# Batch 0's channel product by seven half products too, with w_ch1's quadrants and w_ch2's sums made at other places

## The reference

```
x   = softmax(rot(q) @ rot(k).T / 8) @ v           # heads side by side: 576 x 512 per batch
h   = relu(x.T @ w_tok1) @ w_tok2                  # w_tok1 576 x 256, w_tok2 256 x 576
u   = x + h.T
out = u + relu(u @ w_ch1) @ w_ch2                  # w_ch1 512 x 1536, w_ch2 1536 x 512
```

## Time and profile before

| | |
|---|---|
| time, median of 3 runs | 640.83 us (640.73 to 640.95) |
| profiled execution: span from its first to its last instruction | 639.1 us |
| profiled execution: granted PE clock, mean | 0.998 of full |
| u units of batch 0 begin | at 298.9 us |
| w_ch1 product of batch 0 begins | at 308.6 us |
| u units of batches 1 and 2 begin | at 388.9 and 472.9 us |

### The profile page before, as it was taken

How to read it: one execution, slowest core, us unless ns; L and a number is a source line. 1 busy time by engine, 2 the same in 40 slices (tenths; PEclk the granted TensorE clock), 3 DMA queues, 4 the chain that set the end, 5 groups by cost and what they waited for, 6 DMA issues and landing times.

```text
span 639.1 us, 13808 instructions
## 1 busy us (share of the span) xinstructions
PE 621.5 (97%) x4724; PEld 604.7 (95%) x4724; DVE 509.4 (80%) x877; ACT 464.2 (73%) x1016; POOL 341.0 (53%) x316
## 2 busy tenths in 40 slices
PE   3899999999999999999999999999999999999997
PEld 3799999999999999999999999999999999999997
DVE  6899999999999999987385985569935499553895
ACT  3889999988889899986383664776556765567753
POOL 3999999998888887560900002860017800068200
PEclk9999999999999999999999999999999999999999
DMA  4767766767668774406001332000320002100002
GB/s 133 168 159 197 212 151 179 187 173 183 174 176 211 203 189 114 122 20 216 19 1 44 155 84 75 1 2 2 84 74 0 0 0 80 43 33 1 1 3 74
DMA packets 61898, 63.01 MB, mean 99 GB/s; under 512 B 18896, under 2 KB 46160, under 8 KB 61840
## 3 DMA queue, kind: packets, MB, share of 16 engines
q1 hardware_dynamic: 61392, 62.15, 35.7%
q10 hardware_dynamic: 448, 0.10, 0.1%
HBM read 31.46 MB, written 9.44 MB: 64 GB/s over the span
## 4 chain that ended last, share of the span: by engine, by line
PE 95%; SPq 1%; DVE 1%; DMA 1%; ACT 0%; issue 0%; ACTq 0%; DVEq 0%
PE slot L615 12%; PE rest L648 12%; PE rest L625 9%; PE slot L1344 8%; PE slot L1346 8%; PE slot L1345 8%; PE rest L1344 6%; PE rest L1346 6%; PE rest L1345 6%; PE rest L376 3%; PE rest L576 3%; PE rest L635 2%; PE slot L1376 2%; PE rest L1376 2%; PE rest L224 1%; PE rest L221 1%
## 5 line engine op out<-in xcount | busy, mean ns | idle before, releaser
L1335 POOL TENSOR_TENSOR w_ch_part<-w_ch_sums,w_ch_part 128x512 fp32r<-128x512 f32 x21 | 31.0, 1474 | 173.3 <-ACT w_ch_part L1588 173.3
L984 DVE TENSOR_REDUCE neg_max<-slot 128x1 f32<-128x576 f32 x142 | 106.7, 752 | 6.6 <-PE slot L615 2.2
L1652 ACT ACTIVATE pieces<-h 128x288 fp32r<-128x288 f32 x168 | 73.8, 444 | 49.8 <-PE slot L1346 25.3
L992 DVE TENSOR_TENSOR pt_lo<-rest,pt_hi 128x512 fp32r<-128x512 f32 x144 | 96.0, 677 | 1.9 <-ACT pt_hi L845 1.3
L648 PE MATMUL rest<-pt_hi,v 128*128 128x256 f32 (+1 forms) x320 | 89.3, 303 | 0.0
L845 ACT ACTIVATE pt_hi<-rest 128x512 fp32r<-128x512 f32 x144 | 84.1, 595 | 5.2 <-PE rest L625 4.3
L1743 DVE TENSOR_TENSOR pieces<-h,pieces 128x288 fp32r<-128x288 f32 x168 | 74.6, 454 | 9.4 <-ACT pieces L1652 8.9
L648 PE MATMUL rest<-pt_lo,v 128*128 128x256 f32 (+1 forms) x256 | 69.7, 295 | 0.0
L615 PE MATMUL slot<-key,q_hi 128*128 128x288 f32 x252 | 63.5, 333 | 2.2 <-ACT prob_a L838 1.0
L838 ACT ACTIVATE prob_a<-slot,neg_max 128x576 f32<-128x576 f32 x78 | 58.0, 743 | 10.1 <-DVE neg_max L984 10.0
L648 PEld LDWEIGHTS rest<-pt_hi,v 128*128 128x128 f32 x320 | 60.3, 188 | 0.1
(11 more groups left out here) (263 smaller groups left out, 2107.3 us busy)
## 6 DMA issues: line engine op xcount, KB each, us to landing
key<-t_hi_k SPq DMA_DIRECT2D x31, 144.0 KB, 2.3
key<-t_lo_k SPq DMA_DIRECT2D x31, 144.0 KB, 2.4
raw_qk<-in_q_dram SPq DMA_DIRECT2D x16, 256.0 KB, 2.8
raw_v<-in_v_dram SPq DMA_DIRECT2D x16, 256.0 KB, 3.3
x_scratch<-x_pair SPq DMA_DIRECT2D x16, 256.0 KB, 2.1
stage_or_x<-x_scratch SPq DMA_DIRECT2D x16, 256.0 KB, 4.3
q_hi<-t_hi_q SPq DMA_DIRECT2D x31, 128.0 KB, 2.4
q_cross<-t_hi_q SPq DMA_DIRECT2D x31, 128.0 KB, 2.4
```

Source lines behind the costliest of these rows:

```text
L984: dve.tensor_reduce(neg_max[p % 2][:, i:i + 1], slot[g if 2 <= g < 4 else g % 2][:, :, 0:HALF], AX.XY, ALU.max, negate=True).then_inc(maxe ...
L992: dve.tensor_tensor(pt_lo[:, :, cols], rest[:, bank, :].rearrange("p (j n) -> p j n", j=G), f32(pt_hi[:, 0:G, cols]), ALU.subtract).then_i ...
L1652: act.activation(pieces[:, ring(m), 0, :], source[WEIGHTS[n]][:, ft, :], ACT.Copy).then_inc(piece_hi, 1)
```

## The change

1. Batch 0 uses the seven half products as the other batches do. `hidden`, `hidden_out`, `u_hi`, `u_lo`, `add_u` and the special order of `t1` and `t3` in batch 0 go.
2. w_ch1 is loaded once, by the same eight DMAs, into the places of the quadrants. It is no longer split as a whole. POOL makes the sum S1 and then S3 in late attention (p = 14 and 15), DVE makes S2 at its end and S4 in batch 0. The four loads and the four sums in batch 0's channel stage go.
3. w_ch2's sums move from POOL to DVE, between the steps of the half products; `w2_hi(n)` stands on ACT behind each half product n; of the lo parts, DVE makes numbers 0 and 1 and POOL numbers 2 to 6, behind its 21 ring rests.

The diff, cut to its core:

```diff
 class ChannelWeights:
+    def load(self, sp, w_ch1, n, c):
+        name, c0, col = (("S3", 0, 1), ("A22", CT // 2, 1), ("A11", 0, 0), ("A12", CT // 2, 0))[n]
+        sp.dma_start(self.share[name][:, c, :],
+                     w_ch1[(c0 + c) * P:(c0 + c + 1) * P, col * CH // 2:(col + 1) * CH // 2]).then_inc(self.loaded, 16)
+    def early_sum(self, pool, n):
+        out, x, y, op = (("S1", "S3", "A22", ALU.add), ("S3", "A11", "S3", ALU.subtract))[n]
...
+    def late_sum(self, dve, n):
+        out, x, y = (("S2", "S1", "A11"), ("S4", "A12", "S2"))[n]
...
+        dve.tensor_tensor(self.share[out], self.share[x], self.share[y], ALU.subtract).then_inc(self.late_sums, 1)
# attention, POOL (p = 14, 15) and the end of DVE's list; ACT's eight w1.split_hi go
-                w1.split_lo(pool, p - (N - 2))
+                w1.early_sum(pool, p - (N - 2))
-        w1.split_lo(dve, 2)
+        w1.late_sum(dve, 0)
# mixer, POOL
-        weight_sum("S1", "A21", "A22", ALU.add)
...
+        for k in range(HIDDEN):
+            ring_rest(0, k)
+        for n in range(W2_FIRST, len(WEIGHTS)):      # W2_FIRST = 2
+            w2_lo(n)
# mixer, PE
-                for j in range(PLAIN):
-                    hidden(j)
+            for n in range(len(SHARES)):
+                for i in range(PAIR):
+                    shared(b, n, i)
...
+            if begins and n < W2_FIRST:
+                pe.wait_ge(w2_lo_first, n + 1)
+            elif begins:
+                pe.wait_ge(w2_lo_then, n - W2_FIRST + 1)
# mixer, ACT: ring_part, and shares
+            elif k == 2 and begins:
+                act.wait_ge(x_stored, 48 * PAIRS)
...
+            if k == PAIR and begins:
+                act.wait_ge(w1.early_sums, 2)
+                act.wait_ge(w1.late_sums, 2)
...
                 if n + 2 < len(SHARES):
                     share_part(b, n + 2)
+                if begins:
+                    w2_hi(n)
...
+        ring_part(0, 0, begins=True)
         body(0, begins=True)
# mixer, DVE: shares, and the start of batch 0
             share_rest(b, 2)
+            if begins:
+                w2_sums(0)
+                w2_sums(1)
             for i in range(PAIR):
                 keep(b, i)
+            if begins:
+                w2_sums(2)
             share_rest(b, 3)
+            if begins:
+                w2_sums(3)
             share_rest(b, 4)
+            if begins:
+                w2_lo(0)
             share_rest(b, 5)
...
             share_rest(b, 6)
+            if begins:
+                w2_lo(1)
...
+                first.last_sums(dve)
+                w1.late_sum(dve, 1)
+            shares(b, begins)
```

More of the change, by code:

```diff
@@ L112, in build @@
         with ExitStack() as ctx:
-            then = mixer(nc, ctx, sb, slot, ident, h, h1, pieces, token, wt2, wc1, w1, w1_sums, w1_parts, h_early, x_stored, first, w_ch1, w_ch2,
+            then = mixer(nc, ctx, sb, slot, ident, h, h1, pieces, token, wt2, w1, w1_parts, h_early, x_stored, first, w_ch1, w_ch2,
                          out)
@@ L143 @@
 Mixer = namedtuple("Mixer", "sync gpsimd tensor scalar vector first_token_hi")
+SHARES = ("A11", "S2", "S3", "A22", "A12", "S1", "S4")
 class ChannelWeights:
[L149 to L170, removed]
+    def __init__(self, nc, whole, sums):
+        self.share = {name: sums[:, n] for n, name in enumerate(SHARES)}
+        self.loaded, self.early_sums, self.late_sums = (whole.enter_context(nc.semaphore(f"w_ch1_{n}"))
+                                                        for n in ("loaded", "early_sums", "late_sums"))
@@ L1238, in mixer, with t_count @@
     last_columns = sem("last_columns")
[L1240 to L1245, removed]
+    def t_count(b, which, f):
+        return b * TS + (which - 1) * HF + f + 1
     def used(b, n):
@@ L1279, in sync, with body @@
         sp.dma_start(w2_whole["A21"][:], w[:, top, HC * P:DM]).then_inc(w_in, 16)
[L1281 to L1290, removed]
+        def body(b, last=False):
             if not last:
@@ L1378, in u_unit @@
             mm.then_inc(unit_ready, 1)
[L1380 to L1392, removed]
-                    mm = products(s[:, g, 0:HALF], [w[:, c, ft * P:(ft + 1) * P] for w in wc1],
-                                  [x[:, c, f * HALF:(f + 1) * HALF] for x in ut], c == 0, c == CT - 1)
-            mm.then_inc(unit_ready, 1 if j < PLAIN - 1 else 1 + HIDDEN - PLAIN)
         def shared(b, n, i):
@@ new lines, in body @@
+                first.last_sums(dve)
+                w1.late_sum(dve, 1)
+            shares(b, begins)
+            lo(b, 3)
+            t1(b, 0)
+            lo(b, 4)
+            t1(b, 1)
+            t1(b, 2)
+            lo(b, 5)
+            for f in range(3, HF):
+                t1(b, f)
+                lo(b, 3 + f)
+            for f in range(HF):
+                t2(b, f)
+                lo(b, 9 + f)
+            for f in range(HF):
+                t3(b, f)
+                lo(b, 15 + f)
```

264 lines of the change are left out of this document (78 added, 186 removed).

## The result

The changed kernel takes **663.05 us** (median of five runs, 662.6 to 664.3) where the kernel before takes 640.90 (640.73 to 641.32) beside it: a ratio of **1.0347**, 95% interval 1.0335 to 1.0358, so slower by 3.5%. The forecast was 665.7, with a range of 648 to 672. The profiled execution took 664.3 us, with a span of 662.5; its forecast was 665.7 and 664. A second measurement of the same kernel, in another job, gave 664.33 with a span of 662.4. Two variants of different jobs can therefore differ by some 1.3 us without a cause in the kernel. Two executions far outside the rest, one of 873.82 us of the variant *spread* and one of 2175.91 of the kernel before, are left out everywhere.

What follows compares the result with a forecast made beforehand. PE was taken to bound the kernel, busy 97% of the span and throughout batch 0. The terms -4.8 + 0.8 + 5.0 + 4.0 + 2.15 + 15.9 + 1.8 = +24.9 on 640.83 gave 665.7 us, range 648 to 672.

Steps and rivals of the forecast that it cites:

- Matmuls, -4.8: Batch 0: 36 fewer matmuls at 0.133 us each save 4.8 us.
- Start, +0.8: Start of batch 0: DVE's late w_ch1 sum delays the last normalisation, the store of x and unit 3: +0.8 us.
- Sums in front of keep, +5.0: Before unit 6: two w_ch2 sums on DVE, alternating with POOL's rests, delay DVE's copy of S2: +5.0 us.
- ACT before w2_hi(1), +4.0: Before unit 9: ACT's split of S1 waits for all four w_ch2 sums, holding ring part 9 behind it: +4.0 us.
- Units 12 and 18, 2.15: Later half products: added splits and lo parts delay ring part 12 and POOL's rests; unit 12 waits 1.25, unit 18 0.9 us.
- POOL's five, +15.9: Channel product: POOL's five w_ch2 lo subtractions alternate with DVE's instructions on the shared port, making DVE's lo's late: +15.9 us.
- my 0.4 each: Within POOL's five lo subtractions: 0.4 us for each of four DVE turns, added to 5 x 3.5 us.
- Clock, +1.8: Channel product: after a long wait PE runs at half pace for 3.5 us, once, losing 1.8 us.
- (a): Rival: the stalls are hidden and only the saved matmuls count, 636.0 us; needs keep 0 in time; 5%.
- (b): Rival, channel product: POOL's long subtractions stop DVE's short ones little or not at all, 649.0 us; 18%.
- (c): Rival, channel product: DVE, queued back to back, keeps the port; POOL enters only at gaps; 18.2 for 15.9, so 668; 8%.
- (d): Rival: the clock stays low through the channel product, +23, about 688 us; 4%.

Runs made afterwards that it cites:

- spread: Changed kernel with ACT's splits one half product later, w_ch2's sums and w_ch1's S4 standing apart, all seven lo parts on DVE: 650.91 us, ratio 1.0159.
- the last kernel: Changed kernel without w_ch2's four sums, its seven lo parts written as zeros, POOL's memsets behind DVE's last max: 640.12 us, ratio 0.9985.
- S4 later: Changed kernel with DVE's sum S4 of w_ch1 moved from in front of the share sums to behind w2_lo(0): 664.64 us, ratio 1.0369.
- Splits later: Changed kernel with ACT's splits of w_ch2, except number 0, one half product later: 661.44 us, ratio 1.0321.
- POOL only writes: Changed kernel with POOL's five lo subtractions replaced by ten memsets of the same tiles, which read nothing: 649.53 us, ratio 1.0136.
- lo parts on DVE: Changed kernel with lo parts 2 to 6 moved from POOL to DVE, spread over the channel product: 653.73 us, ratio 1.0196.
- POOL in slices: Changed kernel with each of POOL's five lo subtractions cut into six of 128x256: 661.72 us, ratio 1.0323.
- the first experiment: Changed kernel with POOL's five lo subtractions replaced by ten memsets, with a wait of POOL on itself between them: 649.53 us, ratio 1.0136.

## Why the prediction was right, step by step

- **Matmuls, -4.8**: 4724 less 4688 is 36. Right; the last kernel shows a saving only when nearly everything else is gone.
- **Start, +0.8**: 0.2 before the first unit and 0.4 at unit 3. Right in kind. *S4 later* shows that it is no gain elsewhere.
- **Sums in front of keep, +5.0**: 3.7, by DVE's copy. Two POOL rests were to go ahead of DVE's copy, one in front of sum one and one between the sums; only the second did. ACT made ring part 6 at 316.82, behind `w2_hi(0)`, 1.2 after unit 3 had freed its buffer, so POOL lost a turn and DVE's sum one went first. I had left `w2_hi(0)` out of that chain. A POOL rest is 1.3, the difference. This is read from the rows; no run moved `w2_hi(0)` alone.
- **ACT before w2_hi(1), +4.0**: 2.8, and 1.7 of slow pace ran inside it: without that unit 9 would have waited some 4.4. (The forecast's own terms add up to 24.1, not 24.2.) ACT stood 8.01 before its first S split, released by DVE's sum. *Splits later* confirms the cause.
- **Units 12 and 18, 2.15**: 0.6 at unit 15 and 0.9 at unit 18. Unit 12's 1.25 was swallowed by the slow pace before it; it is there (1.1) in *splits later*, and in *POOL only writes* and *lo parts on DVE*, where no slow pace follows unit 9.
- **POOL's five, +15.9**: the mechanism was right, the size a little high. Piece 2 starts at 369.89, 14.2 after its unstalled 355.70. POOL started at C - 2.5, ahead of max 0, so the last held `lo` is lo 2 and not lo 3. A held `lo` lasts 3.64, not 3.9, and the profile has PE waiting 12.0 ahead of the first pieces, not 14 to 16; the rest of the 14.2 is slow pace and restarts between them. And POOL's five took 17.9 (351.60 to 369.52), not 19.1: from the second on they are spaced 3.6, which is what two of them take with no DVE between the earlier trace rows. The Trainium skill ("Perfetto Trace Analysis", GPSIMD Engine Instruction) would time POOL by such spacings, and this trace agrees: 5 x 3.60 is 18.0 for the 17.9. DVE's turn costs POOL nothing that its own spacing doesn't have, and my 0.4 each was one term too many. An estimate from the slices agrees: (3.51 - 1.30) / 1024 columns is 2.16 ns a column, 0.55 for 256; 0.895 less 0.55 leaves 0.34 for DVE, and 1536 columns make 3.31, so that 3.31 and 0.3 of DVE fit in 3.60.
- **Clock, +1.8**: the term mis-sized the other way. Slow pace was 1.7 after unit 6 (swallowed by the wait at unit 9, as said), 1.7 after unit 9, which I had at nothing, and 2.0 after piece 2: 3.7 that count. The starts are 0.24 apart from 370.29 to 373.50, 333.09 to 335.97 and so on, near half pace, and the granted clock of these stretches, 0.50 in the rows below, is that of the lower level (1.2 GHz); the 0.61 above is a mean over both levels:

```profile
370.30:373.50 3.20, 3.20 (x14) 3.13 (x14) 3.17 (x10) 1.13 (x3) 0.00 (x0) 0.50 0.00 0
333.10:336.20 3.10, 3.10 (x14) 3.10 (x14) 2.66 (x2) 2.84 (x4) 1.74 (x2) 0.50 0.02 5
```

Together: waits of 21.3 where I had 27.9, slow pace of 6.7 where I had 1.8, and a sum of 28.0 for 29.7. So the mechanisms were right, and that the sum came so near is in part luck: the waits were forecast too high (1.7 for POOL's five, 1.3 in front of keep, 1.2 at unit 9), slow pace too low, and the errors took each other back. In POOL's chain 1.2 of the error is my term for DVE's turns and the rest the earlier start; in front of keep it is the order in which two engines' instructions reach the port. Of the 2.7 by which the time lies under the forecast, 1.5 is the profiled span (662.5 for 664); the rest is that the median of the five runs, 663.05, is 1.2 below the profiled one.

Rivals: (a) needed keep 0 in time, and even without w_ch2's sums and lo parts 636 is not reached (640.12). (b) falls with the rows above. (c) is out, since max and `lo` went one by one with POOL, and with writes only it was POOL that kept its row going while DVE's max stood (6.03), the reverse of (c). (d) is out: the pace was back at 373.96.

## What to carry to other kernels

Where one engine is at its bound, its neighbour on a shared port should be idle. Writing alone cost less here (2.2 for 16.2), but it still held DVE's max, and splitting the neighbour's reading finer won 1.9 of 16.2. Before moving work beside a saved product, add up the time that both engines read the shared port in that stretch, with the wait chains over all engines (here DVE's sum, ACT's split, POOL's rest, PE): a wait that is cut at one link comes out at the next. And reckon with slow pace behind each of PE's longer waits, and not once in all, unless another wait follows at once and covers it. It was 1.4 to 3.0 behind every wait of 3 us or more that no other followed. Behind the wait of 2.6 at unit 9 it was 1.7 in the changed kernel and none in *POOL only writes* and *lo parts on DVE*, though up to there they run the same instructions. And in *POOL in slices*, where waits of up to 1.6 follow one another, PE ran at slow pace between them too: the granted clock is 0.50 from 366 to 372.

## What the runs showed of the hardware beyond that

- Who goes next depends on the kind. POOL's subtractions and DVE's instructions take turns one by one (0.895 a pair). POOL's memsets with no wait between them but those on ACT, already met, did not let DVE's one-input max in: it stood through five, 6.03 for 0.46, in the one execution profiled. With a wait of POOL on itself between the memsets (the first experiment) the max got in after one, 1.34 to 1.53. The same row of memsets did nothing to two-input subtractions (0.45 each in the last kernel). That the wait is what lets DVE in was not tried by itself.
- The granted clock can fall some way behind the wait. After unit 9's wait of 2.6 in the changed kernel PE ran nine matmuls at the full pace (331.76 to 332.90) and then at 0.24 from 333.09 on. After the same wait in *POOL only writes* the clock stayed at 1.00:

```profile
331.30:334.00 2.70, 2.70 (x20) 2.70 (x21) 0.95 (x1) 2.70 (x5) 2.34 (x2) 1.00 0.02 6
334.00:337.00 3.00, 2.30 (x18) 2.06 (x16) 1.92 (x2) 3.00 (x7) 2.01 (x1) 1.00 0.00 0
```

What decides between the two cases is not shown.
